# First feed-forward layer, first token tile: from two halves of the tokens with all columns to three parts (half tokens, half columns; other tokens, same columns; all tokens, the other columns)

## The reference, cut to what matters

```
# B, H, S, D = 4, 8, 576, 64; factor = 4; everything float32
q_d, k_d, v_d = mean over groups of 4 positions          # pooled: 144 positions
out_up = repeat(softmax(q_d k_d^T / 8) v_d, 4)           # coarse attention
out_local = softmax(banded scores, |i - j| < 4) v        # 7 neighbours
x = (out_up + out_local) as [2304 tokens, 512]
xn = x / rms(x) * rms_g
y = (silu(xn @ w_gate) * (xn @ w_val)) @ w_out           # 512 -> 1536 -> 512
h = y @ w_in;  out = (s * relu(h)**2 + b) @ w2_out       # 512 -> 2048 -> 512
```

## Time and profile before

| | us |
|---|---|
| median of 3 runs | 1028.01 (1024.22 to 1028.34) |
| the profiled execution's own time | 1027.28 |
| its span, first to last instruction | 1025.2 |
| PE busy | 964.9 (94% of the span) |
| DVE / ACT / POOL busy | 532.1 / 332.3 / 415.3 |

### The profile page before, as it was taken

One profiled execution on the slowest core, in us unless ns is written; L12 is line 12 of the kernel. 1 busy time (PEld: TensorE's weight loads), 2 busy tenths in 40 slices (PEclk: granted clock), 3 DMA queues, 4 the chain that ended last, 5 costly groups with the idle time before them and its releaser, 6 DMA issues.

```text
span 1025.2 us, 13271 instructions
## 1 busy us (share of the span) xinstructions
PE 964.9 (94%) x5080; PEld 782.2 (76%) x5080; DVE 532.1 (52%) x798; ACT 332.3 (32%) x718; POOL 415.3 (41%) x215
## 2 busy tenths in 40 slices
PE   4398899898999999999999999999999999999997
PEld 3276689797777667777777898887888888888896
DVE  4568777875675675555552133343443343333343
ACT  2243565324322341343123244322322232222232
POOL 4788879894886577544630254100000000000000
PEclk9999999999999999999999999999999999999999
DMA  9986347240422132102103233101100200100010
GB/s 252 283 244 195 95 126 223 85 127 19 131 64 84 37 118 77 41 18 70 31 6 123 83 125 103 42 1 42 42 1 6 77 1 1 55 7 1 1 42 21
DMA packets 55290, 79.41 MB, mean 77 GB/s; under 512 B 9852, under 2 KB 38108, under 8 KB 53948
## 3 DMA queue, kind: packets, MB, share of 16 engines
q1 hardware_dynamic: 53212, 73.86, 24.1%
q10 hardware_dynamic: 2016, 4.72, 1.2%
HBM read 67.05 MB, written 11.50 MB: 77 GB/s over the span
## 4 chain that ended last, share of the span: by engine, by line
PE 78%; POOL 7%; DVE 6%; issue 3%; DMA 2%; ACT 2%; SPq 1%; ACTq 0%; POOLq 0%; DVEq 0%
PE bank L717 24%; PE bank L848 6%; PE bank L849 6%; PE bank L850 6%; PE bank L866 6%; PE bank L867 6%; PE bank L868 6%; PE bank L758 4%; PE bank L756 4%; PE bank L757 4%; POOL prod L520 3%; POOL prod L534 2%; DMA rawk<-in_k_dram 2%; PE bank L1481 1%; PE bank L1514 1%
## 5 line engine op out<-in xcount | busy, mean ns | idle before, releaser
L520 POOL TENSOR_TENSOR prod<-qs,ks 128x896 f32<-128x896 f32 x80 | 180.5, 2279 | 77.0 <-DVE sc L540 63.7
L534 POOL TENSOR_TENSOR prod<-sc,vs 128x896 f32<-128x896 f32 x80 | 149.6, 1987 | 56.4 <-DVE x L550 36.8
L887 DVE SCALAR_TENSOR_TENSOR r<-bank,r 128x512 f32<-128x512 f32 (+1 forms) x80 | 51.1, 638 | 183.7 <-ACT r L875 183.7
L850 PE MATMUL bank<-y_h,w2i_l 128*128 128x512 f32 (+1 forms) x320 | 117.7, 368 | 0.0
L717 PE MATMUL bank<-x_h,wv_h 128*128 128x256 f32 (+1 forms) x288 | 104.4, 378 | 8.4 <-DVE h_l L784 7.5
L756 PE MATMUL bank<-h_h,wo_h 128*128 128x256 f32 (+1 forms) x288 | 107.0, 371 | 0.4 <-issue 0.4
L778 DVE TENSOR_TENSOR bank<-bank,u 128x256 f32<-128x256 f32 (+1 forms) x72 | 40.5, 562 | 125.4 <-PE bank L717 119.0
L875 ACT ACTIVATE r<-bank 128x512 f32<-128x512 f32 (+1 forms) x80 | 44.4, 556 | 183.7 <-PE bank L850 183.0
L540 DVE TENSOR_REDUCE sc<-prod 128x14 f32<-128x896 f32 x80 | 85.4, 1078 | 31.4 <-POOL prod L520 31.4
L758 PE MATMUL bank<-h_h,wo_l 128*128 128x256 f32 (+1 forms) x288 | 97.5, 338 | 0.0
L757 PE MATMUL bank<-h_l,wo_h 128*128 128x256 f32 (+1 forms) x288 | 96.8, 336 | 0.0
(11 more groups left out here) (132 smaller groups left out, 1959.0 us busy)
## 6 DMA issues: line engine op xcount, KB each, us to landing
raww<-in_moe_w_out_dram SPq DMA_DIRECT2D x14, 512.0 KB, 3.7
ks<-in_k_dram SPq DMA_DIRECT2D x16, 280.0 KB
vs<-in_v_dram SPq DMA_DIRECT2D x16, 280.0 KB, 4.7
raww<-in_moe_w_in_dram SPq DMA_DIRECT2D x8, 512.0 KB, 3.7
y_raw<-y_scr SPq DMA_DIRECT2D x4, 1024.0 KB, 4.8
out_dram<-o_st SPq DMA_DIRECT2D x16, 256.0 KB, 2.8
rawq<-in_q_dram SPq DMA_DIRECT2D x3, 1152.0 KB, 13.4
rawk<-in_k_dram SPq DMA_DIRECT2D x3, 1152.0 KB, 14.3
```

Of the source, the lines that this page charges most:

```text
L520: pool.tensor_tensor(dst, qv, kv, ALU.mult).then_inc(prod_ready, 1)
L534: pool.tensor_tensor(dst, pv, vv, ALU.mult).then_inc(prod_ready, 1)
L850: last = pe.matmul(o, w2i_l[:, m, kk, :], y_h[t % 2][:, kk, 0:w], start=False, stop=kk == DT - 1)
```

## The change

Tile 0 becomes three parts. Part 0 is tokens 0 to 255 with column blocks 0 to 5; part 1 is tokens 256 to 511 with the same blocks; part 2 is all 512 tokens with blocks 6 to 11. That is 6 + 6 narrow steps and 6 wide ones, s 0 to 17; tile 1 begins at s = 18. The four sums of `out1` for tile 0 lie in four banks of 512 columns, in which the halves share the bank, and are stored once, as those of the other tiles. In part 0 and part 2 the gate has one bank (`gate(s)` waits for `silu(s-1)`), in part 1 two. The turning of x for tile 1 moves from steps 8 to 10 of the second chunk to the places it has in the other tiles: round 0 at the end of step 16, the rest within step 17.

The order of pieces is new (out 2 comes before gate 3), and so are all places by hand. POOL gets pieces 5, 7, 9 after qk products 4, 7, 12 and pieces 11, 13, 15, 17 after pv products 1, 4, 8, 11. DVE's `add_pooled` moves to steps 13 and 15, ACT's `squares` to 14 and 15. On SP, loads for tile 2 and of v windows stand between the pieces.

```diff
+MH = M1 // 2
+FIRST_ORDER = []
+for _g in range(2):
+    _j = _g * MH // 2
+    FIRST_ORDER += [("gate", _j), ("val", _j)]
+    for _j in range(_g * MH // 2 + 1, (_g + 1) * MH // 2):
+        FIRST_ORDER += [("gate", _j), ("val", _j), ("out", _j - 1)]
+    FIRST_ORDER += [("out", (_g + 1) * MH // 2 - 1)]
...
+HI_AT = {0: (6, 7), 2: (8,), 4: (9,), 5: (10,), 6: (11,), 7: (12,), 9: (13,), 10: (14,), 12: (15,), 13: (16,), 14: (17,)}
+LO_AT = {0: (4,), 2: (6,), 4: (8,), 8: (10,), 11: (12,), 13: (14,), 14: (16,)}
+QK1_AT = {1: (6, 7), 3: (8,), 4: (9,), 5: (10, 11), 6: (12, 13), 7: (14, 15)}
+PV1_AT = {10: (0,), 11: (1, 2), 12: (3, 4, 5, 6), 13: (7, 8, 9, 10), 14: (11, 12, 13), 15: (14, 15)}
+
+REST_AT = {("qk", 4): (5,), ("qk", 7): (7,), ("qk", 12): (9,), ("pv", 1): (11,), ("pv", 4): (13,), ("pv", 8): (15,), ("pv", 11): (17,)}
...
+PARTS = [(0, 0, 0, 256, range(MH)), (1, 0, 256, 256, range(MH)), (1, 0, 0, W_, range(MH, M1))]
+PARTS += [(t + 1, t, 0, CHUNKS[t + 1][2], range(M1)) for t in range(1, TILES)]
+STEP = [(p, m) for p in range(len(PARTS)) for m in PARTS[p][4]]
...
-ROUND_AT = ((2, 11), (3, 10), (4, 10))
+ROUND_AT = ((1, 11), (2, 11), (3, 10), (4, 10))
...
         def gate(pe, s):
-            wait(pe, u_ready, s - 1 if 0 < s < 2 * M1 else s)
+            p, m = STEP[s]
+            wait(pe, u_ready, s - 1 if MH < s <= 2 * MH else s)
...
         def silu(act, s):
-            wait(act, hf_ready, s - 1 if w < W_ and m else s)
+            wait(act, hf_ready, s - 1 if w < W_ and (m or p == 1) else s)
...
@@ sync: order of loads
             load_piece(sp, 13)
+            load_qk(sp, 2, 0)
+            load_qk(sp, 2, 1)
             load_piece(sp, 14)
-            load_qk(sp, 1, 7)
+            load_ct(sp, 1)
             load_piece(sp, 15)
+            load_v(sp, 1, 2)
             load_piece(sp, 16)
+            load_v(sp, 1, 3)
             load_piece(sp, 17)
...
@@ gpsimd
             for n in range(16):
-                if n == 6:
-                    weight_lo(pool, 5)
-                if n == 8:
-                    weight_lo(pool, 7)
...
                 qk_mult(pool, 1, n)
-            weight_lo(pool, 15)
+                for i in REST_AT.get(("qk", n), ()):
+                    weight_lo(pool, i)
...
                 for n in range(16):
                     pv_mult(pool, a, n)
+                    if a == 1:
+                        for i in REST_AT.get(("pv", n), ()):
+                            weight_lo(pool, i)
...
@@ scalar, in the step loop
-                if c == 1 and m == 3:
+                if s == 14:
                     squares(act, 1, 0)
-                if c == 1 and m == 5:
-                    squares(act, 1, 1)
-                if c == 1 and m == 6:
+                if s == 16:
                     normalise(act, (0, 1), 2)
...
                 hidden_hi(act, s)
+                if s == 15:
+                    squares(act, 1, 1)
+                if s == 16:
+                    normalise(act, (2, 3), 2)
...
@@ vector, in the step loop
-                for n in PV1_AT.get((c, m), ()):
-                    pv_reduce(dve, 1, n)
-                if c == 1:
-                    if m == 2:
+                    for n in PV1_AT.get(s, ()):
+                        pv_reduce(dve, 1, n)
+                    if s == 13:
                         add_pooled(dve, 1, 0)
-                    if m == 4:
+                    if s == 15:
                         add_pooled(dve, 1, 1)
-                    if m == 5:
                         inverse_root_of(dve, 1)
```

More of the change, by code:

```diff
@@ L644, in xt_bank @@
         def xt_bank(c, r):
-            if c > 2 or r % 2 == 0:
-                return XT[0]
-            return XT[1] if c == 0 else bank[7]
+            return XT[1] if c == 0 and r else XT[0]
         def transpose_x(pe, c, r):
@@ L653, in transpose_x @@
             pe.wait_ge(xn_ready, 2 if c == 0 else FAC * (t + 1))
-            wait(pe, xl_done, n_round if c > 2 else n_round - 1)
-            if c == 1 and r == 1:
-                pe.wait_ge(co_ready, 2 * B)
+            wait(pe, xl_done, n_round if c else n_round - 1)
+            if c == 2 and r == 0:
+                pe.wait_ge(u_ready, 2 * MH)
             per = W_ // w
@@ L747, in out1 @@
         def out1(pe, s):
-            c, m = divmod(s, M1)
-            w = CHUNKS[c][2]
+            p, m = STEP[s]
+            c, t, col0, w, ms = PARTS[p]
             pe.wait_ge(hl_ready, s + 1)
             if m == 0:
-                wait(pe, y_evac, DT * c)
+                wait(pe, y_evac, DT * t)
             for dt in range(DT):
-                o = sums_of(c, dt)
+                o = YB[dt][:, col0:col0 + w]
                 cols = slice(dt * P, (dt + 1) * P)
-                pe.matmul(o, wo_h[:, m, cols], h_h[:, s % 3, 0:w], start=m == 0 and not (c < 2 and dt % 2), stop=False)
+                pe.matmul(o, wo_h[:, m, cols], h_h[:, s % 3, 0:w], start=m == 0 and p != 1, stop=False)
                 pe.matmul(o, wo_h[:, m, cols], h_l[:, s % 3, 0:w], start=False, stop=False)
-                last = pe.matmul(o, wo_l[:, m, cols], h_h[:, s % 3, 0:w], start=False, stop=m == M1 - 1 and not (c < 2 and dt % 2 == 0))
+                last = pe.matmul(o, wo_l[:, m, cols], h_h[:, s % 3, 0:w], start=False, stop=m == M1 - 1)
             last.then_inc(y_step, 1)
         def silu(act, s):
-            c, m = divmod(s, M1)
-            w = CHUNKS[c][2]
+            p, m = STEP[s]
+            w = width(s)
             act.wait_ge(gate_done, s + 1)
-            wait(act, hf_ready, s - 1 if w < W_ and m else s)
+            wait(act, hf_ready, s - 1 if w < W_ and (m or p == 1) else s)
             act.activation(u[:, u_part(s)], gate_bank(s)[:, 0:w], ACT.Silu).then_inc(u_ready, 1)
         def hidden_hi(act, s):
-            w = CHUNKS[s // M1][2]
+            w = width(s)
             act.wait_ge(hf_ready, s + 1)
@@ L784, in hidden_lo, with store_y, copy_y @@
             dve.tensor_tensor(h_l[:, s % 3, 0:w], VB[s % 2][:, 0:w], f32(h_h[:, s % 3, 0:w]), ALU.subtract).then_inc(hl_ready, 1)
[L786 to L805, removed]
+        def store_y(act, t):
+            w = WIDTH2[t]
+            act.wait_ge(y_step, TILE_END[t])
+            wait(act, y_stored, 16 * t)
+            for dt in range(DT // 2 if t == TILES - 2 else DT):
+                act.activation(y_st[t % 2][:, dt, 0:w], YB[dt][:, 0:w], ACT.Copy).then_inc(y_evac, 1)
+            act.wait_ge(y_evac, DT * (t + 1))
+            act.dma_start(y_scr[t][:, :, 0:w], y_st[t % 2][:, :, 0:w]).then_inc(y_stored, 16)
+        def copy_y(dve, t):
+            w = WIDTH2[t]
+            dve.wait_ge(y_step, TILE_END[t])
+            wait(dve, y_stored, 16 * t)
             for dt in range(DT // 2, DT):
-                dve.tensor_copy(y_st[t % 2][:, dt, col0:col0 + w], YB[dt][:, 0:w]).then_inc(y_evac, 1)
+                dve.tensor_copy(y_st[t % 2][:, dt, 0:w], YB[dt][:, 0:w]).then_inc(y_evac, 1)
         def load_y(sp, t):
             w = WIDTH2[t]
-            sp.wait_ge(y_stored, 16 * (chunk_of_tile(t) + 1))
+            sp.wait_ge(y_stored, 16 * (t + 1))
             if t == 0:
@@ L1025, in _ @@
             load_piece(sp, 12)
+            load_qk(sp, 1, 7)
             load_piece(sp, 13)
+            load_qk(sp, 2, 0)
+            load_qk(sp, 2, 1)
             load_piece(sp, 14)
-            load_qk(sp, 1, 7)
+            load_ct(sp, 1)
             load_piece(sp, 15)
+            load_v(sp, 1, 2)
             load_piece(sp, 16)
+            load_v(sp, 1, 3)
             load_piece(sp, 17)
[L1032 to L1037, removed]
+            for h in range(4, H):
+                load_v(sp, 1, h)
+            for a in range(2, TILES):
+                for h in range(2, H):
+                    load_qk(sp, a, h)
+                load_v(sp, a, 0)
+                load_v(sp, a, 1)
                 if a + 1 < TILES:
```

131 lines of the change are left out of this document (52 added, 79 removed).

## The result

The change makes the kernel slower by 1.1%: 1037.66 us median of 7 runs (1035.16 to 1041.42), against 1028.01 for the kernel before on the same chip (7 runs, 1023.02 to 1029.98). The ratio is 1.0108, 95% interval [1.0076, 1.0139]. A second measurement of the changed kernel as it is (e8, 4 runs beside the experiments) gave 1038.88 us (1038.31 to 1039.69) and a ratio of 1.0125 [1.0106, 1.0144]. That is 14.1 us above the kernel before in its own series (1024.82), where 10 to 13 had been expected. The forecast was 1043, range 1034 to 1048.

What follows compares the result with a forecast made beforehand. PE and POOL were taken to be full at once from 202 to 236 us. The shift of +15.2 us on the profiled 1027.3 gave 1042.5, and 0.7 for the median made 1043; range 1034 to 1048.

Steps and rivals of the forecast that it cites:

- Step 1: Product 5 and the start: split 5 ahead of product 5 delays `gate(2)` to 158.6, 4.3 us wait plus 1.65 of clock.
- Step 2: POOL's qk products: ten products, two splits and 7.6 us of waits end at 191.8; pv product 0 starts at 203.2.
- Step 3: POOL's pv products: four added splits (10.6 us) and waits for v and ACT; last product ends at 250.0, before 234.0.
- both late steps are mild: Rival: POOL waits for neither v nor ACT, or the early delay is absorbed; 1035.5 to 1037 us; chance 0.19.
- Step 4: Last pv product to tile 1: 12.0 us to 262.0, PE waits 11.6; tile 1 starts 276.3, its fourth step 300.9.
- The sum: Tile 1's fourth step at 300.9 against 285.7 by the same additions over the old orders: shift +15.2 us.
- PE's own gain: Twelve narrow steps (51.0 us) become six wide ones (49.2): 1.8 us less, hidden under PE's wait.
- tile 2 too: Rival: POOL reaches tile 2's products 16 us late, adding up to 5 us, 1048; chance 0.08.
- The other side: Rival: PE's gain is real, x ready in time, tile 1's fourth step 15.1 us sooner, 1013; chance 0.10 in whole or part.

Runs made afterwards that it cites:

- e8: A second measurement of the changed kernel as it is, 4 runs beside the experiments: 1038.88 us, ratio 1.0125.
- e1: The changed kernel with POOL's split of piece 5 behind qk product 5 again instead of product 4: 1029.8 us, ratio 1.0055.
- e4: The kernel before with POOL's split of piece 5 ahead of qk product 5 instead of product 6: 1028.92 us, ratio 1.0034.
- e2: e1 with ACT's high part of piece 17 made in step 13 instead of 14: 1030.35 us, ratio 1.0047.
- e3: The changed kernel with the low parts of pieces 11, 13, 15, 17 left out, plain copies by ACT in their place: 1028.01 us, ratio 1.0029.
- e6: The changed kernel, three parts kept, with splits, high parts, reductions and loads put in another order: 1028.72 us, ratio 1.0025.
- e9: e6 with the load of tile 1's key and query 7 moved ahead of a store and the load of ct: 1023.71 us, ratio 0.9981.
- e10: e9 with the splits of pieces 15, 16 and 17 on DVE instead of POOL: 1021.83 us, ratio 0.9974.
- e5: The changed kernel with the low parts of pieces 11, 13, 15, 17 on DVE instead of POOL: 1033.3 us, ratio 1.0087.

## Why the prediction was right

Sign, time and mechanism held: PE trades four waits for one long one, made by POOL's later end. By its steps:

- **Step 1** held: `gate(2)` at 158.12 with 3.86 us of wait (forecast 158.6 and 4.3), behind this queue on DVE, which answers to the earlier trace rows:

```profile
153.97 1.09 DVE L551 TENSOR_REDUCE sc<-prod 128x14 f32<-128x896 f32 x1 [6.18 <-POOL prod L531]
154.97 0.42 DVE L782 TENSOR_TENSOR bank<-bank,u 128x256 f32<-128x256 f32 x1
```

  e1 shows its price by removal and e4 by addition. The price was 5 to 6 us in my expectation and 7.9 in the run (5.9 against e8); the products' waits for DVE in steps 3 to 5 hang on it too.
- **Step 2**: pv product 0 at 200.83, forecast 203.2. Two sizes were off against each other. Waits for the reductions were 6.51 + 2.45 + 1.06 = 10.0 where I had 7.6; but each product took 2.12 us, not 2.5 (the mean of the earlier trace rows mixes products of 2.1 and of 3.1 us). From the end of product 15 (190.59) to pv product 0 it was 10.2 us where I had 11.4. On DVE in between, the split of piece 10 took 3.14 us, not 2.1, and the softmax maximum (195.90 to 197.04) 1.1, not 3.4.
- **Step 3**: last pv product ends at 241.46 + 7.21 = 248.67, forecast 250.0. Four splits took 2.44 + 2.40 + 3.34 + 3.06 = 11.2 (forecast 10.6), v 2.13 (1.6), the closed wait for piece 17 4.60 (4.5). That wait was sized right and not worth its length: without it (e2) the fourth step moves 1 us, less than two profiles of one kernel differ. The gap of up to 6 us between the forecast and "both late steps are mild" was therefore not there to be had at that place. Nor did the splits' 11 us cost 11: without them and the wait, 15.8 us, the fourth step moves 9.6 (7.5 against e8; e3), since the reductions' places by step hold POOL next.
- **Step 4**: 12.9 us from there to the turning (forecast 12.0); wait of PE 12.68 (11.6). Tile 1 starts 12.0 us after the turning and not 14.3, since the 3.0 us for splits behind each turning did not come (PE's waits there sum to 0.3); the fourth step 25.6 later, not 24.6. The clock, priced at 1.65 us behind each wait, was under-sized: it was 0.50 over 158 to 163, with PE busy 4.88 us, and 0.50 over 261 to 266, with 4.40, so by half of these times some 2.4 and 2.2 us (my estimate from these two rows). Together 299.18 for 300.9.
- **The sum**: +14.5 for +15.2, with errors that cancel in steps 2 and 4, so its closeness is in part luck; the second profile (+12.4) is 2.8 off. The time is 5.3 us under the forecast, and the shift accounts for 0.7 of this. The rest I put down to differences between executions: the profiled run is itself 3.4 us above the median of its kernel (1041.05 and 1037.66), its seven runs lie in 1035.2 to 1041.4, and the clock at the later handover fell in one profile and not in the other. The medians differ by 9.7 us in this series and by 14.1 in that of e8, against 15 forecast. From the profile before plus the median's distance such a spread can't be foreseen; the range held it.
- **PE's own gain** was put at 1.8 us. In the three kernels with the new places and the clock of before, PE is busy 1.6 (e6), 2.3 (e9) and 3.05 us (e10) less. In the change it was hidden behind PE's wait as forecast.

Of the rivals, "tile 2 too" did not happen: the span's difference is smaller than the shift. "The other side" put the point of balance at a last pv product ending at 234 (87.6 behind `gate(0)`). That point was placed too late. e6 (86.5) should have been a little faster and is slower by 0.25%; e9 (81.5) should have gained 6 us and its fourth step comes 2.1 us sooner. The fourth step stands 50.5 us behind that end in the change, as in the sum (50.9), but 55.2 in e6 and e9 and 53.7 in e10, so that stretch is no constant once the end comes sooner. The 15 us of gain were never reached: with x ready in time (e10) PE still waits 9.0 us for the small engines.

What stays open: e8's shift is 2.1 us smaller than that of the same kernel's first profile. In e8 pv product 0 starts 1.4 us sooner behind `gate(0)`, with a clock of 0.66 over 158 to 163 instead of 0.50, and POOL waits 0.85 us for v instead of 2.13; 0.8 us of that is lost again behind the turning. Why clock and transfer differ between two executions is not shown. The parts that e3 and e5 price overlap with step 1, which they keep; no run took both away.

## What to carry to other kernels

When engines run fixed orders that are tied together by step numbers, a wait seen at one place is seldom worth its length: take it away in thought and look at what stands next in the same step (e2 got some 1 of 4.6 us), but look as hard for the one place that holds a whole group back (e1: one split moved by one product, 5.9 to 7.9 us; e9: one load moved ahead of two other transfers, 5.0 us). A restructuring that gives one engine work and another one ease must be judged after its places have been chosen anew: the same three parts gave +1.1% with the first places and -0.3% with the last. And read the chain to the point where the engine that bounds picks it up; in five of these kernels it was a constant 13 us behind POOL's last product, and in e6, e9 and e10, where that product ended sooner, 16.5 to 16.8.

## What the runs showed of the hardware

- A DVE operation on 128x4 elements, 0.16 us alone, lasted 2.26, 2.02 and 1.95 us beside POOL's tensor operations, each until the POOL instruction at hand had ended (e9), and 0.17 with POOL idle (e10). Not only operations with two tensor inputs did so: L629 and L630 are tensor-scalar operations with one. L631, a tensor-scalar operation on integers, took 0.15 between them; it follows L630 with no semaphore between the two and falls where one POOL product ends and the next begins, so these runs do not tell whether its type or its place spared it. I had not counted on this for work so small: a chain of 13 such operations went from 2.3 to 8.1 us.

  The Trainium skill (SBUF — State Buffer, section "SBUF: two separate sides") has one pair of ports locked for a whole instruction, either by a GpSimd operation or by a DVE operation that has two SBUF inputs (against a GpSimd operation that reads SBUF) or runs in a 2-port perf mode; the later one waits. The two-input operation at L633 agrees with it (1.95 us). For L629 and L630, with one input, it would take the perf mode, and no run here shows in which mode they ran.
- Behind the same 2.4 us of PE idle at the later handover, the granted clock was 1.00 over 590 to 600 in one profile of the changed kernel and 0.67 over 590 to 595 in the other (e8). Behind 12.7 us of idle it was at the 1.2 GHz level over 261 to 266 (0.50) and 0.99 over the next 5 us.
- The first layer's gate step starts at 142.5 to 146.4 us in eleven profiles, and at 143.0 and 142.5 in two kernels (e3, e5) whose code up to there is that of the change (145.9 and 145.2). A difference of 3 us between two profiles ahead of the change is no effect of it, so stages are compared from a mark behind it.
